# One turn for the last 64 keys of two heads, and one limit operation per beat

## The chip, the cores and the metric

The kernel runs on one core of one Trainium2 chip. The time is the device time in microseconds (us) of one execution; the kernel before took 1011.58 us (median of three runs, 1011.28 to 1013.16). In the text PE is TensorE, DVE is VectorE, ACT is ScalarE, POOL is GpSimd and SP is SyncE.

## The reference

```python
scores = scale * (q @ k.T)                      # 4 batches, 8 heads, 576 tokens, head size 64
thresh = scores.max(-1) - tau
scores = where(scores >= thresh, scores, -1e9)  # all far below a row's maximum is dropped
attn = exp(scores - scores.max(-1)); attn /= attn.sum(-1) + 1e-9
x = (attn @ v) put together over heads           # 2304 tokens x 512
x = (s * relu(x @ w_in)**2 + b) @ w_out          # first layer, hidden size 2048
h = x @ w_in2; x = (h * sigmoid(1.702 * h)) @ w_out2    # second layer
```

All is fp32. The kernel splits operands into a high and a low part of a faster fp32 format (fp32r) and adds the products of the parts.

## The kernel before

**Work and order.** The attention is cut into 160 tiles of query rows (128 or 96 rows each, 576 keys). Two tiles make a beat; there are 80 beats. Each engine has its own program, a loop over beats, with an order written out by hand; semaphores tie the engines together. From beat 15 on the steps of the first layer are woven in (one step per beat), and after the attention the steps and then the second layer (`TWINS`) follow alone.

**One beat.** PE computes the scores of the even tile (`scores_of`, four matmuls into one of two PSUM buffers), then those of the odd one. DVE makes the scaled row minimum (`row_max`, line 1045, which writes back the scaled scores and is followed by a read of the accumulator), then `limit_of` (line 1052: minimum plus tau, one column), per tile. In between DVE has `context_lo`, `invert_pair` (line 1059, the reciprocal of two row sums of the previous beat) and, from beat 16, `gated`. ACT computes exp (`exponent`, line 1269) as soon as the minimum is there. DVE then masks the even tile and the odd tile (`mask`, line 1071), with `gated_lo` (line 1108) between them in later beats. POOL adds eps (line 1547), and in its next beat scales both tiles (`norm`, line 1554). The scores buffer is free for PE again when its tile is masked.

**Turning the probabilities.** The products with the values need the keys on partitions. For the first six groups (32 tiles, beats 0 to 15) PE turns them two beats later: `turn_tile` has four transposes of 128 keys (line 769) into `y_ps[0]` or `y_ps[1]`, and one of the last 64 keys (line 773) into `y_ps[2]`, at column 0 for the even tile and column 128 for the odd one. ACT copies the four blocks (`copy_main`) and, once for both tiles, the last 64 keys (`copy_tails`, line 1301, 64 partitions). On PE a beat reads: scores even, turn even, scores odd, turn odd. For all later tiles DVE turns blocks of 32x32 (`turn`, line 1085) and DMAs put them in place; those are not touched by the change. `context_of` multiplies with the values: five chunks of 128 keys for each of two heads, where the fifth chunk has 64 keys and 64 rows of zeros.

**Ends of waits.** A tile's slot in `prob` (four slots) is free for `exponent` when PE has turned the tile. `context_hi` (line 1279, ACT) and `context_lo` (line 1093, DVE) split the result of `context_of` into its parts.

Of the kernel before, what the change touches and what calls it, by code (L numbers as in the profile page):

```python
# [9 lines left out]
ALU = mybir.AluOpType  # L10
ACT = mybir.ActivationFunctionType

P = 128
# [9 lines left out]
BATCH, HEADS_PER_BATCH, SEQ, HEAD_DIM = 4, 8, 576, 64  # L23
HEADS = BATCH * HEADS_PER_BATCH
PAIRS_PER_BATCH = HEADS_PER_BATCH // 2
# [2 lines left out]
BLK = 32  # L28
BLOCKS = SEQ // BLK
KEY_CHUNKS = 5  # L30
EPS = 1e-9
STATS = 8
PROBS = 4
# [19 lines left out]
PE_GROUPS = LONE_GROUPS + 2  # L53
FIRST_TILE = [2 * sum(TILES_PER_HEAD[n] for _, _, _, n in GROUPS_OF[:w]) for w in range(len(GROUPS_OF) + 1)]
FIRST_BEAT = [tile // 2 for tile in FIRST_TILE]
TILES = FIRST_TILE[-1]
# [163 lines left out]
B_FROM = 75  # L220
A_FROM = 88
A_APART = 4

# [28 lines left out]
PIECES = pieces_in_order()  # L254
# [56 lines left out]
VALUES = value_loads()  # L311
# [3 lines left out]
def tiles_of(beat, lag=0):  # L315
    return range(2 * beat - lag, 2 * beat - lag + 2)
# [41 lines left out]
def build(nc, q, k, v, consts_in, ident_in, slabs, twin_in, twin_out, out):  # L358
    ctx = ExitStack()
    with ctx:  # L360
# [7 lines left out]
        tau_in, s_c, b_c, eps_c, scale_c, tau_c, lower_c = (consts[:, n:n + 1] for n in range(7))  # L368
        ident = sbuf(ctx, "ident", [P, P])
# [64 lines left out]
        prob = sbuf(attn, "prob", [P, PROBS, SEQ])  # L434
        blocks = sbuf(attn, "blocks", [P, 2, BLOCKS, 2 * TILES_PER_HEAD[LONG], BLK])
        prob_t = sbuf(attn, "prob_t", [P, KEY_CHUNKS, 2 * LONG])
        neg_max = sbuf(attn, "neg_max", [P, STATS])
        limit = sbuf(attn, "limit", [P, STATS])
# [26 lines left out]
        y_ps = [ctx.enter_context(nc.psum_tensor(f"y_ps{n}", [P, 512], F32)) for n in range(GROUPS)]  # L465
# [6 lines left out]
        pads_zeroed = sem("pads_zeroed")  # L472
# [10 lines left out]
        max_ready = sem("max_ready")  # L483
# [50 lines left out]
        def turned_rows(w):  # L534

            return early_t if w < LONE_GROUPS and w % 2 == 1 else prob_t

        def turned_column(w, side, q):

            if w < LONE_GROUPS:  # L540
                return LONG * side + q
            return LONG * half_of(w) + SHORT * side + q
# [192 lines left out]
        def _(pe):  # L735
# [23 lines left out]
            def turn_tile(j):  # L759

                m = rows_of(j)
                w, side, t = TILE_AT[j]
                if j == 0:
                    pe.wait_ge(ident_loaded, 16)
                pe.wait_ge(normed, j + 1)
                if j >= 2:
                    pe.wait_ge(main_copied, j - 1)
                for c in range(KEY_CHUNKS - 1):
                    nc.tensor.transpose(y_ps[j % 2][:, c * P:c * P + m], prob[0:m, j % PROBS, c * P:(c + 1) * P],
                                        ident[0:m, 0:m])  # L770
                if side == 0 and j > 0:
                    pe.wait_ge(tail_copied, j // 2)
                nc.tensor.transpose(y_ps[2][0:64, side * P:side * P + m],
                                    prob[0:m, j % PROBS, (KEY_CHUNKS - 1) * P:SEQ], ident[0:m, 0:m]
                                    ).then_inc(rows_pe_turned, 1)

            def context_of(piece):

                w, n, _ = PIECES[piece]
                quads = (2 * n, 2 * n + 1) if is_long(w) else (0, 1, 2)  # L780
                if w >= PE_GROUPS:
                    for a in quads:
                        half = moved_into(w, a)
                        pe.wait_ge(moved[half][a], 64 * moves_before(w + 1, half, a))
                elif rides(piece):
                    pe.wait_ge(tail_copied, FIRST_BEAT[w + 1])
                    pe.wait_ge(main_copied, FIRST_TILE[w + 1])
                else:
                    pe.wait_ge(tail_copied, FIRST_BEAT[w] + n + 1)
                    pe.wait_ge(main_copied, FIRST_TILE[w] + 2 * n + 2)  # L790
                    pe.wait_ge(pads_zeroed, 2)
                    if piece > 0:
                        pe.wait_ge(context_lo_ready, piece)
                i = VALUE_OF[piece]
                pe.wait_ge(v_loaded[i % 2], 16 * (i // 2 + 1))
                for c in range(KEY_CHUNKS):
                    for side in range(2):
                        place = piece_bank(piece)[64 * side:64 * side + 64, :]
                        if w >= PE_GROUPS:
                            start = LONG * (n if is_long(w) else half_of(w))  # L800
                            rows = prob_t[:, c, start:start + LONG].rearrange("p (a s q) -> p a s q", a=len(quads),
                                                                              s=2)[:, :, side, :]
                            place = place.rearrange("p (a q) -> p a q", a=len(quads))
                        else:
                            start = turned_column(w, side, P * n)
                            rows = turned_rows(w)[:, c, start:start + piece_size(piece)]
                        mm = nc.tensor.matmul(place, v_sb[:, i % 2, side, c, :], rows,  # L807
                                              start=(c == 0), stop=(c == KEY_CHUNKS - 1))
                mm.then_inc(context_ready, 1)
# [208 lines left out]
        def _(dve):  # L1018
# [27 lines left out]
                                        accum_out=neg_max[0:m, j % STATS:j % STATS + 1]  # L1046
                                        ).then_inc(max_ready, 1)

            def limit_of(j):
                m, r = rows_of(j), j % STATS  # L1050
                dve.wait_ge(max_ready, j + 1)
                nc.vector.tensor_scalar(limit[0:m, r:r + 1], neg_max[0:m, r:r + 1], tau_c[0:m, :], None, ALU.add
                                        ).then_inc(limit_ready, 1)

            def invert_pair(j):
# [5 lines left out]
            def mask(j):  # L1061

                m, r = rows_of(j), j % STATS
                dve.wait_ge(limit_ready, j + 1)
                dve.wait_ge(exp_ready, j + 1)
                if j % 2 == 1 and riding(j // 2) is not None:
                    dve.wait_ge(context_hi_ready, riding(j // 2) + 1)
                if j % 2 == 0 and turn_due(j // 2 - MLP_FROM) is not None:
                    dve.wait_ge(x_ready, turns_by(j // 2 - MLP_FROM))
                p = prob[0:m, j % PROBS, :].rearrange("p (a n) -> p a n", a=2)  # L1070
                nc.vector.scalar_tensor_tensor(  # L1071
                    out=p, in0=scores[j % 2][0:m, :, 0:HALF], scalar=limit[0:m, r:r + 1],
                    in1=p, op0=ALU.is_le, op1=ALU.mult,
                    accum_out=row_sum[0:m, r:r + 1]).then_inc(masked, 1)
# [22 lines left out]
            def gated(n):  # L1097

                dve.wait_ge(gate_ready, n + 1)
                g = gate[:, n % 2, :]  # L1100
                nc.vector.scalar_tensor_tensor(out=g, in0=h_bank(n)[:, 0:TOK], scalar=s_c, in1=g, op0=ALU.mult,  # L1101
                                               op1=ALU.mult).then_inc(square_ready, 1)
# [80 lines left out]
            for beat in range(BEATS):  # L1183
                s = beat - MLP_FROM
                for j in tiles_of(beat):
                    if j < TILES:
                        row_max(j)
                        limit_of(j)
                    if j % 2 == 0 and alone(beat - 1) is not None:
                        context_lo(alone(beat - 1))  # L1190
                    if j % 2 == 0 and 0 <= j - 2 < TILES:
                        invert_pair(j - 2)
                    if j % 2 == 0 and s >= 1:
                        gated(s - 1)
                for j in tiles_of(beat):
                    if j < TILES:
                        mask(j)
                    if j % 2 == 0 and s >= 2:
                        gated_lo(s - 2)
                if riding(beat) is not None:  # L1200
                    context_lo(riding(beat))
                for j in tiles_of(beat, 2):
                    if PE_TILES <= j < TILES:
                        turn(j)
# [39 lines left out]
        def _(act_eng):  # L1244
# [48 lines left out]
            def copy_tails(j):  # L1293

                m = rows_of(j)
                w, _, t = TILE_AT[j]
                first, end = turned_column(w, 0, 0), 2 * turned_column(w, 1, 0) - turned_column(w, 0, 0)
                act_eng.wait_ge(rows_pe_turned, j + 2)
                if j == FIRST_TILE[w] and w >= 2:
                    act_eng.wait_ge(context_ready, TILES_PER_HEAD[LONG] * min(w - 1, LONE_GROUPS - 1))  # L1300
                nc.scalar.copy(turned_rows(w)[0:64, KEY_CHUNKS - 1, first:end].rearrange("p (s q) -> p s q", s=2)
                               [:, :, t * m:(t + 1) * m],
                               y_ps[2][0:64, 0:2 * P].rearrange("p (s q) -> p s q", s=2)[:, :, 0:m]
                               ).then_inc(tail_copied, 1)

            def slab_in_hi(n):

# [394 lines left out]
```

## Time and profile before

| what | value |
|---|---|
| median of three runs | 1011.58 us |
| the profiled execution | 1009.4 us, of which its span 1007.6 us |
| PE busy | 993.2 us (99%) |
| DVE, POOL, ACT busy | 798.0, 657.9, 606.6 us |
| TensorE clock granted | full over the span |

The profile counts an engine as busy while an instruction of it runs. Matmuls are pipelined and overlap, and their ends are modelled, so that a busy PE can still be a little late. In the timeline a name such as `scores<-k_hi,q_hl` is output and inputs; square brackets give the idle time of the engine ahead of the row and what ended it. Starts are us from the start of the span.

### The profile page before, as it was taken

How to read it: one execution, taken by the hardware profiler on the slowest of the kernel's cores; microseconds unless marked ns; L12 is line 12 of the kernel's file. 1: busy time of each engine (PE TensorE's matmuls, PEld its weight loads, DVE VectorE, ACT ScalarE, POOL GpSimd, SP SyncE). 2: the span in 40 equal slices, each digit the busy share in tenths (PEclk: the TensorE clock that was granted, in tenths of full speed). 3: DMA queues.
4: the chain of work that ended last, by engine and by line, in shares of the span. 5: the costliest groups of instructions: out<-in, count | busy, mean ns of one | idle time of the engine just before them, and what ended most of it. 6: DMA issues, size and time to landing. Idle time of an engine off the chain costs nothing.

```text
span 1007.6 us, 18212 instructions
## 1 busy us (share of the span) xinstructions
PE 993.2 (99%) x5922; PEld 895.4 (89%) x5922; DVE 798.0 (79%) x1749; ACT 606.6 (60%) x1124; POOL 657.9 (65%) x713
## 2 busy tenths in 40 slices
PE   8999999999999999999999999999999999999998
PEld 7788888888888888888899999998989989899897
DVE  7989999999999999999547766877767776566663
ACT  7877666666676666765555755555546555454443
POOL 6769997778788888886657775454544545445452
PEclk9999999999999999999999999999999999999999
DMA  7236776897977797778733541112122221222212
GB/s 216 73 116 187 209 204 189 218 239 213 228 199 191 204 246 190 209 179 217 211 106 126 185 150 32 63 42 85 44 82 87 102 84 46 81 87 102 84 48 79
DMA packets 97581, 142.50 MB, mean 141 GB/s; under 512 B 10320, under 2 KB 68944, under 8 KB 97488
## 3 DMA queue, kind: packets, MB, share of 16 engines
q1 hardware_dynamic: 97488, 141.34, 48.7%
q8 instruction: 49, 0.80, 0.3%
q14 instruction: 44, 0.36, 0.1%
HBM read 102.96 MB, written 4.72 MB: 107 GB/s over the span
## 4 chain that ended last, share of the span: by engine, by line
PE 85%; DVE 11%; issue 1%; DMA 1%; ACT 1%; POOL 0%; SPq 0%; DVEq 0%; POOLq 0%; ACTq 0%
PE shared L831 12%; PE y_ps L850 11%; PE shared L924 10%; PE y_ps L948 10%; PE scores L948 10%; PE scores L924 8%; PE scores L745 7%; PE scores L807 7%; PE scores L831 5%; PE y_ps L870 5%; DVE scores L1045 4%; DVE prob L1071 3%; PE scores L870 2%; DVE blocks L1085 1%; DMA k_raw<-k 1%
## 5 line engine op out<-in xcount | busy, mean ns | idle before, releaser
L1269 ACT ACTIVATE prob<-scores,neg_max 128x576 f32<-128x576 f32 (+1 forms) x160 | 118.6, 742 | 122.5 <-DVE scores L1045 122.4
L1614 POOL TENSOR_TENSOR a_sum_lo<-a_sum,a_hi 128x256 fp32r<-128x256 f32 x96 | 70.1, 740 | 182.5 <-DVE scores L1167 123.9
L1560 POOL TENSOR_TENSOR w_lo<-w_raw,win_hi 128x512 fp32r<-128x512 f32 x96 | 129.1, 1345 | 22.1 <-ACT win_hi L1311 17.7
L1567 POOL TENSOR_TENSOR w_lo<-w_raw,wout_hi 128x512 fp32r<-128x512 f32 x96 | 126.5, 1318 | 23.4 <-ACT wout_hi L1318 23.4
L1045 DVE TENSOR_SCALAR_CACHE_REDUCE scores<-scores,consts 128x576 f32<-128x576 f32 (+1 forms) x160 | 129.5, 809 | 13.1 <-PE scores L745 11.7
L1554 POOL TENSOR_SCALAR prob<-prob,row_inv 128x576 f32<-128x576 f32 (+1 forms) x160 | 126.8, 805 | 6.1 <-DVE row_inv L1059 5.7
L1071 DVE SCALAR_TENSOR_TENSOR prob<-scores,limit,prob 128x576 f32<-128x576 f32 (+1 forms) x160 | 128.1, 808 | 0.3
L831 PE MATMUL shared<-act_hi,win_hi 128*128 128x384 f32 x280 | 94.8, 339 | 1.1 <-DVE gate L1101 0.9
L831 PE MATMUL shared<-act_hi,w_lo 128*128 128x384 f32 x280 | 94.3, 337 | 0.0
L831 PE MATMUL shared<-act_lo,win_hi 128*128 128x384 f32 x280 | 93.9, 335 | 0.0
L1085 DVE STREAM_TRANSPOSE blocks<-prob 128x576 f32<-128x576 f32 (+1 forms) x128 | 91.4, 751 | 1.9 <-DMA prob_t<-blocks 1.7
L1108 DVE SCALAR_TENSOR_TENSOR g_lo<-gate,consts,g_hi 128x384 fp32r<-128x384 f32 x96 | 92.7, 966 | 0.2 <-ACT g_hi L1332 0.2
L1179 DVE TENSOR_TENSOR g_lo<-gate,g_hi 128x384 fp32r<-128x384 f32 x96 | 62.2, 650 | 33.4 <-ACT g_hi L1403 32.8
L745 PE MATMUL scores<-k_hi,q_hl 128*128 128x288 f32 (+1 forms) x320 | 76.6, 320 | 6.8 <-DVE prob L1071 6.2
L1332 ACT ACTIVATE g_hi<-gate,consts 128x384 fp32r<-128x384 f32 x96 | 59.0, 614 | 38.8 <-PE y_ps L870 27.9
L1395 ACT ACTIVATE gate<-scores 128x384 f32<-128x384 f32 x48 | 23.6, 492 | 94.9 <-DVE scores L1167 94.9
L1403 ACT CAST g_hi<-gate 128x384 fp32r<-128x384 f32 x96 | 49.2, 514 | 49.4 <-DVE gate L1174 40.0
L850 PE MATMUL y_ps<-wout_hi,g_hi 128*128 128x512 f32 x192 | 75.6, 394 | 0.0
L850 PE MATMUL y_ps<-wout_hi,g_lo 128*128 128x512 f32 x192 | 75.5, 393 | 0.0
L807 PE MATMUL scores<-prob_t,v_sb 128*64 128x192 f32 x800 | 73.8, 331 | 1.5 <-DVE prob L1071 0.9
L850 PE MATMUL y_ps<-w_lo,g_hi 128*128 128x512 f32 x192 | 74.9, 390 | 0.0
L1532 POOL TENSOR_TENSOR q_hl<-q_raw,q_hl 128x384 fp32r<-128x384 f32 (+1 forms) x51 | 49.0, 961 | 37.7 <-DVE g_lo L1108 31.2
(157 smaller groups left out, 2956.6 us busy)
## 6 DMA issues: line engine op xcount, KB each, us to landing
w_raw<-slabs SPq DMA_DIRECT2D x93, 512.0 KB, 4.2
a_raw<-twin_in SPq DMA_DIRECT2D x24, 512.0 KB, 4.6
o_raw<-twin_out SPq DMA_DIRECT2D x24, 512.0 KB, 3.6
prob_t<-blocks SPq DMA_DIRECT2D x96, 120.0 KB, 2.8
k_raw<-k SPq DMA_DIRECT2D x32, 288.0 KB, 4.6
prob_t<-blocks SPq DMA_DIRECT2D x96, 96.0 KB, 2.9
v_sb<-v SPq DMA_DIRECT2D x26, 320.0 KB, 4.3
q_raw<-q SPq DMA_DIRECT2D x40, 192.0 KB, 4.4
```

The costliest lines, as they stand in the source:

```text
L745: mm = nc.tensor.matmul(scores[j % 2][0:m, half, 0:HALF], q_hl[i % Q_RING][:, q0:q0 + m], part[key_slot(e)][:, half * HALF:(half + 1) * HALF],
L807: mm = nc.tensor.matmul(place, v_sb[:, i % 2, side, c, :], rows, start=(c == 0), stop=(c == KEY_CHUNKS - 1))
L831: mm = nc.tensor.matmul(bank[:, 0:TOK], wp[:, w], act_at(xp, c, tile * TOK, TOK), start=(c == 0 and k == 0), stop=(c == DC - 1 and k == 2))
L850: mm = nc.tensor.matmul(y_ps[g][:], gp[:, n % 2, toks], wp[:, :], start=(f == 0 and k == 0), stop=(f == SLABS - 1 and k == 2))
L924: mm = nc.tensor.matmul(twin_bank(x), wp, xp, start=(c == 0 and k == 0), stop=(c == 1 and k == 2))
L948: mm = nc.tensor.matmul(z_bank(tile, g), gp[:, i, toks], wp, start=(e == 0 and i < 2 and k == 0), stop=(e == TWIN_SLABS - 1 and i >= 2 and ...
L1045: nc.vector.tensor_scalar(place, place, scale_c[0:m, :], None, ALU.mult, ALU.min, accum_out=neg_max[0:m, j % STATS:j % STATS + 1]).then_in ...
L1071: nc.vector.scalar_tensor_tensor(out=p, in0=scores[j % 2][0:m, :, 0:HALF], scalar=limit[0:m, r:r + 1], in1=p, op0=ALU.is_le, op1=ALU.mult, ...
L1269: nc.scalar.activation(prob[0:m, j % PROBS, :].rearrange("p (a n) -> p a n", a=2), scores[j % 2][0:m, :, 0:HALF], ACT.Exp, bias=neg_max[0: ...
L1554: nc.gpsimd.tensor_scalar(prob[0:m, j % PROBS, :], prob[0:m, j % PROBS, :], row_inv[0:m, r:r + 1], 1.0, ALU.mult, ALU.mult).then_inc(norme ...
L1560: nc.gpsimd.tensor_tensor(in_of(w_lo, n), in_of(w_raw, n), win_hi[n % IN_HI][:].bitcast(F32), ALU.subtract).then_inc(win_lo_ready, 1)
L1567: nc.gpsimd.tensor_tensor(out_of(w_lo, n), out_of(w_raw, n), wout_hi[n % OUT_HI][:].bitcast(F32), ALU.subtract).then_inc(wout_lo_ready, 1)
```

## The change

For the tiles that PE turns, the odd head's keys are rolled by 64 columns on the host, so that its last 64 keys stand first in its slot of `prob`, right behind the last 64 of the even head in the slot before. One transpose over these 128 adjacent columns turns both; it stands behind the four transposes of the even tile and waits for the odd tile's `norm` too. The values of the odd head have their fifth chunk in partitions 64 to 127 and zeros in 0 to 63, and for the even head the reverse, so that both heads multiply the same turned columns. For the tiles that DVE turns, keys and values of the odd head are rolled alike. `copy_tails` copies 128 partitions by half the columns. And DVE makes both limits of a beat in one operation, after `gated` and both `row_max`.

```diff
-                    nc.tensor.transpose(y_ps[j % 2][:, c * P:c * P + m], prob[0:m, j % PROBS, c * P:(c + 1) * P],
-                                        ident[0:m, 0:m])
-                if side == 0 and j > 0:
-                    pe.wait_ge(tail_copied, j // 2)
-                nc.tensor.transpose(y_ps[2][0:64, side * P:side * P + m],
-                                    prob[0:m, j % PROBS, (KEY_CHUNKS - 1) * P:SEQ], ident[0:m, 0:m]
-                                    ).then_inc(rows_pe_turned, 1)
+                    mm = nc.tensor.transpose(y_ps[j % 2][:, c * P:c * P + m],
+                                             prob[0:m, j % PROBS, TAIL * side + c * P:TAIL * side + (c + 1) * P],
+                                             ident[0:m, 0:m])
+                if side == 0:
+                    pe.wait_ge(normed, j + 2)
+                    if j > 0:
+                        pe.wait_ge(tail_copied, j // 2)
+                    first = (j % PROBS + 1) * SEQ - TAIL
+                    mm = nc.tensor.transpose(y_ps[2][:, 0:m],
+                                             prob[0:m, :, :].rearrange("p a n -> p (a n)")[:, first:first + 2 * TAIL],
+                                             ident[0:m, 0:m])
+                mm.then_inc(rows_pe_turned, 1)
...
-                            start = turned_column(w, side, P * n)
+                            start = turned_column(w, side if c < KEY_CHUNKS - 1 else 0, P * n)
...
-            def limit_of(j):
+            def limit_pair(j):
                 m, r = rows_of(j), j % STATS
-                dve.wait_ge(max_ready, j + 1)
-                nc.vector.tensor_scalar(limit[0:m, r:r + 1], neg_max[0:m, r:r + 1], tau_c[0:m, :], None, ALU.add
+                dve.wait_ge(max_ready, j + 2)
+                nc.vector.tensor_scalar(limit[0:m, r:r + 2], neg_max[0:m, r:r + 2], tau_c[0:m, :], None, ALU.add
                                         ).then_inc(limit_ready, 1)
...
-                dve.wait_ge(limit_ready, j + 1)
+                dve.wait_ge(limit_ready, j // 2 + 1)
...
                     if j < TILES:
                         row_max(j)
-                        limit_of(j)
...
                     if j % 2 == 0 and s >= 1:
                         gated(s - 1)
+                if 2 * beat < TILES:
+                    limit_pair(2 * beat)
...
-                act_eng.wait_ge(rows_pe_turned, j + 2)
+                q0 = turned_column(w, 0, t * m)
+                act_eng.wait_ge(rows_pe_turned, j + 1)
+                if j == 0:
+                    act_eng.wait_ge(pads_zeroed, 2)
...
-                nc.scalar.copy(turned_rows(w)[0:64, KEY_CHUNKS - 1, first:end].rearrange("p (s q) -> p s q", s=2)
-                               [:, :, t * m:(t + 1) * m],
-                               y_ps[2][0:64, 0:2 * P].rearrange("p (s q) -> p s q", s=2)[:, :, 0:m]
-                               ).then_inc(tail_copied, 1)
+                nc.scalar.copy(turned_rows(w)[:, KEY_CHUNKS - 1, q0:q0 + m], y_ps[2][:, 0:m]).then_inc(tail_copied, 1)
...
+    keys[1::2] = np.roll(keys[1::2], TAIL, axis=2)
```

## Rows read from the trace of the kernel before

**Rows 1.** The chain that ended last, shares of the span by engine.

```profile
PE 85%; DVE 11%; issue 1%; DMA 1%; ACT 1%; POOL 0%; SPq 0%; DVEq 0%; POOLq 0%; ACTq 0%
```

**Rows 2.** Busy us by stretch: length, PE, PEld, DVE, ACT, POOL; clock, DMA share, GB/s.

```profile
14.00:67.00 53.00, 47.45 (x478) 41.39 (x479) 50.19 (x155) 45.00 (x94) 38.68 (x57) 1.00 0.35 109
...
83.00:132.00 49.00, 47.50 (x285) 41.38 (x282) 48.43 (x121) 33.42 (x62) 45.65 (x48) 1.00 0.70 197
132.00:184.00 52.00, 51.49 (x325) 45.30 (x325) 50.27 (x128) 33.13 (x61) 41.85 (x50) 1.00 0.74 204
184.00:485.00 301.00, 300.91 (x1950) 264.82 (x1948) 287.96 (x721) 198.27 (x374) 243.52 (x274) 1.00 0.81 210
```

**Rows 3.** Timeline of beat 7: start us, us, engine, line, operation, tiles.

```profile
34.87 0.83 DVE L1045 TENSOR_SCALAR_CACHE_REDUCE scores<-scores,consts 128x576 f32<-128x576 f32 x1 [0.15 <-PE scores L745]
...
35.48 0.43 PE L745 MATMUL scores<-k_lo,q_hl 128*128 128x288 f32 x2
35.58 0.29 ACT L1279 CAST act_hi<-shared 128x128 fp32r<-128x128 f32 x1
35.61 0.14 DVE L1045 DVE_READ_ACCUMULATOR scores<-scores,consts 128x1 f32 x1
...
35.78 0.21 DVE L1052 TENSOR_SCALAR limit<-neg_max,consts 128x1 f32<-128x1 f32 x1
35.91 0.28 DVE L1093 TENSOR_TENSOR act_lo<-shared,act_hi 128x128 fp32r<-128x128 f32 x1
...
36.11 0.16 DVE L1059 RECIPROCAL row_inv<-row_sum_eps 128x2 f32<-128x2 f32 x1
...
36.18 0.81 DVE L1045 TENSOR_SCALAR_CACHE_REDUCE scores<-scores,consts 128x576 f32<-128x576 f32 x1
...
36.49 0.37 ACT L1301 COPY early_t<-y_ps 64x256 f32<-64x256 f32 x1
...
37.09 0.21 DVE L1052 TENSOR_SCALAR limit<-neg_max,consts 128x1 f32<-128x1 f32 x1
37.22 0.81 DVE L1071 SCALAR_TENSOR_TENSOR prob<-scores,limit,prob 128x576 f32<-128x576 f32 x1
37.31 1.47 POOL L1554 TENSOR_SCALAR prob<-prob,row_inv 128x576 f32<-128x576 f32 x2
...
37.95 0.81 DVE L1071 SCALAR_TENSOR_TENSOR prob<-scores,limit,prob 128x576 f32<-128x576 f32 x1
...
38.09 0.54 PE L745 MATMUL scores<-k_hi,q_hl 128*128 128x288 f32 x2 [0.33 <-DVE prob L1071]
...
38.93 0.82 DVE L1045 TENSOR_SCALAR_CACHE_REDUCE scores<-scores,consts 128x576 f32<-128x576 f32 x1 [0.15 <-PE scores L745]
39.05 0.11 PEld L773 LDWEIGHTS y_ps<-ident,prob 128*64 128x64 f32 x1
```

**Rows 4.** Timeline of beat 3, the tail's transpose and the norm before it.

```profile
17.79 1.48 POOL L1554 TENSOR_SCALAR prob<-prob,row_inv 128x576 f32<-128x576 f32 x2
...
18.98 0.11 PEld L773 LDWEIGHTS y_ps<-ident,prob 128*64 128x64 f32 x1
...
19.93 0.83 DVE L1045 TENSOR_SCALAR_CACHE_REDUCE scores<-scores,consts 128x576 f32<-128x576 f32 x1
```

**Rows 5.** Timeline of beat 21, with the first layer woven in.

```profile
102.12 0.78 DVE L1045 TENSOR_SCALAR_CACHE_REDUCE scores<-scores,consts 96x576 f32<-96x576 f32 x1
...
103.13 0.15 DVE L1059 RECIPROCAL row_inv<-row_sum_eps 128x2 f32<-128x2 f32 x1
...
104.33 1.77 POOL L1554 TENSOR_SCALAR prob<-prob,row_inv 96x576 f32<-96x576 f32 x2
...
104.75 0.80 DVE L1071 SCALAR_TENSOR_TENSOR prob<-scores,limit,prob 96x576 f32<-96x576 f32 x1
...
105.48 1.02 DVE L1108 SCALAR_TENSOR_TENSOR g_lo<-gate,consts,g_hi 128x384 fp32r<-128x384 f32 x1
```

**Rows 6.** Groups by line and shape from 75 to 485 us: busy us, mean ns.

```profile
L1108 DVE SCALAR_TENSOR_TENSOR g_lo<-gate,consts,g_hi 128x384 fp32r<-128x384 f32 x63 | 43.9, 697 | 0.0
```

More of the change, by code:

```diff
@@ L30 @@
 KEY_CHUNKS = 5
+TAIL = 64
 EPS = 1e-9
@@ L1296, in copy_tails @@
                 w, _, t = TILE_AT[j]
-                first, end = turned_column(w, 0, 0), 2 * turned_column(w, 1, 0) - turned_column(w, 0, 0)
-                act_eng.wait_ge(rows_pe_turned, j + 2)
+                q0 = turned_column(w, 0, t * m)
+                act_eng.wait_ge(rows_pe_turned, j + 1)
+                if j == 0:
+                    act_eng.wait_ge(pads_zeroed, 2)
                 if j == FIRST_TILE[w] and w >= 2:
                     act_eng.wait_ge(context_ready, TILES_PER_HEAD[LONG] * min(w - 1, LONE_GROUPS - 1))
-                nc.scalar.copy(turned_rows(w)[0:64, KEY_CHUNKS - 1, first:end].rearrange("p (s q) -> p s q", s=2)
-                               [:, :, t * m:(t + 1) * m],
-                               y_ps[2][0:64, 0:2 * P].rearrange("p (s q) -> p s q", s=2)[:, :, 0:m]
-                               ).then_inc(tail_copied, 1)
+                nc.scalar.copy(turned_rows(w)[:, KEY_CHUNKS - 1, q0:q0 + m], y_ps[2][:, 0:m]).then_inc(tail_copied, 1)
             def slab_in_hi(n):
@@ L1676 @@
         queries.append(np.concatenate([cols, cols], axis=0))
-    keys = k_t.reshape(HEADS, HEAD_DIM, SEQ)
-    values = np.zeros((BATCH, HEADS_PER_BATCH, KEY_CHUNKS * P, HEAD_DIM), np.float32)
-    values[:, :, 0:SEQ, :] = v
-    values = values.reshape(BATCH, PAIRS_PER_BATCH, 2, KEY_CHUNKS, P, HEAD_DIM).transpose(0, 1, 4, 2, 3, 5)
-    values = np.stack([values[key] for key, _, _ in VALUES])
+    keys = k_t.reshape(HEADS, HEAD_DIM, SEQ).copy()
+    keys[1::2] = np.roll(keys[1::2], TAIL, axis=2)
+    values = np.zeros((2, BATCH, PAIRS_PER_BATCH, 2, KEY_CHUNKS * P, HEAD_DIM), np.float32)
+    values[:, :, :, :, 0:SEQ, :] = v.reshape(BATCH, PAIRS_PER_BATCH, 2, SEQ, HEAD_DIM)
+    values[1, :, :, 1, SEQ:SEQ + TAIL, :] = values[1, :, :, 1, SEQ - TAIL:SEQ, :]
+    values[1, :, :, 1, SEQ - TAIL:SEQ, :] = 0.0
+    values[0, :, :, 1, 0:SEQ, :] = np.roll(values[0, :, :, 1, 0:SEQ, :], TAIL, axis=2)
+    values = values.reshape(2, BATCH, PAIRS_PER_BATCH, 2, KEY_CHUNKS, P, HEAD_DIM).transpose(0, 1, 2, 5, 3, 4, 6)
+    values = np.stack([values[int(PIECES[first][0] < PE_GROUPS)][key] for key, first, _ in VALUES])
     first, second = slabs_of(moe_w_in, moe_w_out)
```

## The prediction, made before the changed kernel was run

> **What bounds the kernel now.** I read the chain of waits first, then busy time by stretch, then the timeline of single beats. The chain gives PE 85% and DVE 11% [rows 1]. The stretches place DVE's share: from 14 to 67 us (beats 2 to 14, attention alone) DVE is busy 50.19 of 53 us and PE 47.45; from 83 to 132 us (8 beats, with the first layer woven in) DVE is busy 48.43 of 49 us and PE is idle 1.50; from 132 to 184 us PE is idle 0.51; from 184 to 485 us only 0.09 of 301 us [rows 2]. Behind 485 us there is no line of the change. So DVE time is worth something up to about 184 us, and PE time behind that; a us won early moves all of PE's later work up by a us, because PE has no idle time later in which it could be lost.
>
> In an attention beat the loop is: mask of the even tile starts 37.22, PE's next scores start 38.09, the next row minimum 38.93, that is 1.71 us; then from the row minimum of the even tile at 34.87 to its mask at 37.22 are 2.35 us. Period 4.06 us, all through DVE [rows 3]. Within it: row minimum even 34.87, accumulator read to 35.75, limit 35.78, `act_lo` 35.91, reciprocal 36.11, row minimum odd 36.18, limit 37.09, mask 37.22 [rows 3].
>
> **The change part by part.**
>
> *One limit less.* The even tile's limit goes in all 80 beats. It starts 0.03 behind the end of the accumulator's read (35.75 to 35.78) and the next operation 0.13 behind its start, so `act_lo` starts 1.04 behind the row minimum [rows 3]. What follows a row minimum with no wait the trace does not show. From above: it starts when the read ends, at 0.88. From below: it starts with the read, at 0.74 (the odd mask starts 0.73 behind the even one, across a read, 37.22 to 37.95). In between: the limit (0.21 long) is followed after 0.13 and the reciprocal (0.16) after 0.07, so the next one starts 0.08 to 0.09 ahead of the end; by that it starts at 0.80 [rows 3]. I take 0.80, a saving of 0.24 (bounds 0.16 and 0.30).
>
> *What is late next.* The odd tile's row minimum would then start at 0.80 + 0.27 = 1.07 instead of 1.31. The odd tile's scores end at 35.91, 1.04 behind the even row minimum [rows 3], and the wait for them costs DVE some 0.03 more, as its own waits do (35.75 to 35.78 above). With the wider weight load below that is about 1.09. So in these beats 0.22 is saved, not 0.24, and no more than that even by the lower bound.
>
> *The pair's limit in front of the mask.* Before, the mask of the even tile waits for nothing that is late: it starts 0.13 behind the odd tile's limit, which it does not need. Now it needs this very operation: 0.21 of length and the 0.03 seen from the read's end to the limit's start [rows 3], 0.24 to 0.25, so 0.12 later. Below, nothing is lost if the hand-over costs no more than an ordinary start; above, 0.2 if it costs a good half again. I take 0.12. Net 0.10 a beat in attention beats, where DVE alone is late; where the odd row minimum waits for another engine, the beat gets 0.12 longer or, with slack at the mask, stays. The operation itself has two columns for one; nothing.
>
> The Trainium skill ("VectorE: DVE Perf Modes", The DRAIN you can't avoid) says that the next operation never starts before the pipe is empty, and that a semaphore between two operations therefore costs nothing extra. By that rule the mask would not be 0.12 later and a beat would gain 0.22. The rows disagree: an operation that does not wait starts 0.08 ahead of the end of the one before, one that waits 0.03 behind it [rows 3].
>
> *Attention beats 2 to 14.* ACT holds `act_lo` back in some: in beat 7 `act_hi` ends at 35.87, `act_lo` starts at 35.91 [rows 3], behind a cast of keys. By the order of the splits in the code this is so in beats 4, 6 and 7, and in beat 14 behind a cast of weights. There the removed limit gives nothing, and the mask's 0.12 is taken up, since the next even row minimum may be 0.12 later without `act_lo` being later. Seven beats (5, 8 to 13) gain 0.10: 0.7 us. Beats 2 and 3 have no `act_lo`; their odd row minimum waits for scores, so each may lose up to 0.12, and I take 0.15 for both.
>
> *The joint transpose.* Each pair loses one transpose, 16 in all, behind the odd tile's scores, where PE waits for the mask anyway (0.33 idle at 38.09 [rows 3]): worth nothing. The joint one has 128 columns for 64 in its weight load, about 0.03 longer, in front of the odd tile's scores: counted above. It now waits for the odd tile's `norm`; behind it on PE stand the odd tile's scores, and DVE waits for those. In beat 8 the norms end at 38.78 and the tail's load stands at 39.05: 0.27 of slack, in a beat where POOL had split keys [rows 3]. In beat 3 the norms end at 19.27 and the load stood at 18.98 [rows 4]: 0.29 too late. POOL's chain there starts behind a reciprocal that itself stands behind a removed limit and comes up to 0.24 earlier. I take 0.08 lost, once; bounds 0 and 0.3.
>
> *The copy of the tails.* It is 128 x 128 in place of 64 x 256 (0.37 [rows 3]); `act_hi` with 128 x 128 takes 0.29. ACT has idle time ahead of the odd exp, and the copy's wait ends a turn earlier. Nothing.
>
> Attention stretch: 0.7 - 0.15 - 0.08 = 0.5 us gained (bounds: 0.3 lost, 0.8 gained).
>
> *Woven beats.* Beat 16 waits for PE between its row minima: no gain, and the limit's 0.12 hides behind a later wait for `act_hi`. Beat 17 and the 8 beats from 83 to 132 us are DVE's throughput: row minimum 102.12, reciprocal 103.13, mask 104.75 [rows 5]. The row minimum is 0.78 here, so reciprocal, `gated` and odd minimum come 0.24 earlier, the mask 0.12: 9 x 0.12 = 1.1 us (bounds 9 x 0.04 and 9 x 0.18, the latter 1.6). PE has 1.50 us idle to give from 83 to 132 [rows 2], so 1.1 fits. `gated` being 0.24 earlier also ends PE's short waits for it.
>
> *Beats 25 to 33.* PE idles 0.51 us [rows 2], some of it for DMA. I take 0.4 (0.1 to 0.5). Behind that 0.09 is left: nothing.
>
> **The sum.** 0.5 + 1.1 + 0.4 = 2.0 us. The profiled execution of 1009.4 us (span 1007.6 and 1.8 around it) would come to 1007.4; it lies 2.2 under the median of the runs, which would come to 1009.6. The sum's own bounds are -0.3 + 0.4 + 0.1 = 0.2 and 0.8 + 1.6 + 0.5 = 2.9 us: 1011.4 to 1008.7.
>
> **Rivals.**
> 1. *The wait costs nothing (the skill's rule above as a mechanism here).* Beats gain 0.22 to 0.24: 7 x 0.22 - 0.08 = 1.5, then 1.5 (all of PE's idle time to 132 us) and 0.5: 3.5 us, 1008.1. Against it stand the starts in [rows 3].
> 2. *The end is elsewhere.* The odd row minimum waits in every attention beat for scores behind the joint transpose, and in the woven beats POOL, busy 45.65 of 49 us [rows 2], takes DVE's place through `norm`. For it: the scores end only 0.03 before the new start. Then 0.3 is lost first and perhaps 0.6 won later: 1011.3, no change that can be told from noise.
> 3. *Slower: DVE runs into POOL.* `gated_lo` takes 1.02 us beside a `norm` (104.33, 1.77 long; its two take 1.47 at 37.31) [rows 3, 5], and its mean over the woven beats is 0.697 [rows 6]. The mask moves against POOL's order, and `gated_lo` with it. If it fell beside the norms in every beat, a beat would be 0.32 longer on DVE: 9 x 0.32 = 2.9 lost before 132 us against 1.1 won, and behind that DVE, which has 301 - 287.96 = 13 us idle to 485 us [rows 2], would be late in some of its 46 beats, about 1.5 us more. With the 0.5 won: 2.8 us slower, 1014.4. It decides from the point where the mean rises by 0.12, what a beat wins. Against it: the move is only 0.1 to 0.2, and nothing says that it goes to the worse side.
>
> **How the numbers follow.** Forecast 0.57, rival 1 0.12, rival 2 0.18, rival 3 0.13. About 0.2% (2 us) is what a measurement here can tell from no change. The forecast lies on that edge and gives 0.33 to faster, 0.24 to the same; rival 1 goes to faster, rival 2 to the same, but for 0.01, rival 3 to slower. Faster 0.45, same 0.41, slower 0.14. The range reaches a little past rival 1 (PE's restarts after idle time may go too, which no term holds) and less than half of the way from rival 2 to rival 3: 1007.4 to 1012.6.
>
> **What would show it.** Right: line 1052's successor 80 times, the odd row minimum 1.07 to 1.12 behind the even one in beats 8 to 13 and its mask 0.24 to 0.25 behind the limit's start; a period of 3.96 there; beat 26 about 1.6 us earlier; from 184 us on all of PE's starts shifted by one constant, about 2 us. Wrong: the operation behind the even row minimum starts at 0.88 or waits; PE's joint load waits for POOL in more than beat 3; `gated_lo` above 0.75 in the mean; or PE's shift shrinks between 184 and 485 us.

## The result and the profile after

The changed kernel takes 1018.32 us (median of 6, 1017.13 to 1019.50) against 1010.63 (median of 6, 1009.16 to 1013.16) for the kernel before on the same chip: ratio 1.0082, interval 1.007 to 1.0094. It is 7.7 us slower. The forecast was 1009.6 us with a range to 1012.6; both are wrong, and so is the sign.

The profiled execution took 1019.28 us (span 1017.5 and 1.8 around it), 9.9 more than that of before. The chain that ended last, by engine, answers to [rows 1]: DVE's share went from 11% to 17%.

```profile
PE 74%; DVE 17%; DMA 3%; issue 2%; SPq 2%; ACT 1%; POOL 0%; DVEq 0%; POOLq 0%; ACTq 0%
```

Busy time in the same stretches as [rows 2] (length, then PE, PEld, DVE, ACT and POOL busy with their counts; clock, DMA share, GB/s):

```profile
14.00:67.00 53.00, 42.93 (x425) 38.02 (x425) 49.16 (x131) 39.52 (x86) 35.66 (x53) 0.97 0.35 108
...
83.00:132.00 49.00, 46.50 (x283) 40.03 (x282) 48.43 (x113) 34.30 (x64) 43.93 (x47) 1.00 0.66 191
132.00:184.00 52.00, 51.52 (x324) 45.46 (x323) 50.35 (x119) 33.31 (x60) 42.81 (x50) 1.00 0.68 191
184.00:485.00 301.00, 297.71 (x1916) 262.14 (x1915) 286.63 (x667) 198.27 (x370) 241.04 (x272) 1.00 0.80 208
```

DVE has fewer operations in every row and is hardly less busy: from 83 to 132 us 113 in place of 121, both times 48.43 us. So its operations got longer. PE's idle time from 184 to 485 us went from 0.09 to 3.29 us. Where the time was lost is seen in the starts of the even row minima, before and after: beat 2 14.86 and 14.87; beat 4 22.69 and 24.77; beat 8 38.93 and 41.25; beat 14 63.15 and 67.80; beat 34 184.54 and 190.10; beat 79 478.56 and 487.87. That is +2.1 in beats 2 and 3, +0.2 to beat 8, +2.3 from 8 to 14, +0.9 to beat 34, +3.8 to beat 79, and 0.6 after it.

The operation that got longer is the one that the change made. Before, a limit is one column, and never takes more than 217 ns; after, it is two columns (views of one line's instructions: count, ns of the shortest, median and longest, first and last start). The first fence is of before, the second of after; the last line of the second is the reciprocal, which had two columns before too.

```profile
L1052 DVE TENSOR_SCALAR limit<-neg_max,consts x160: 208/214/217, 7.9 to 481.2; 128x1 f32<-128x1 f32 x96, 96x1 f32<-96x1 f32 x64
```

```profile
L1062 DVE TENSOR_SCALAR limit<-neg_max,consts x80: 224/544/831, 8.9 to 490.2; 128x2 f32<-128x2 f32 x48, 96x2 f32<-96x2 f32 x32
...
L1069 DVE RECIPROCAL row_inv<-row_sum_eps x80: 119/158/166, 11.6 to 494.6; 128x2 f32<-128x2 f32 x80
```

Half as many limits take 40.8 us (mean 510 ns) where 160 took 34.0. The timeline of beat 9 after the change shows what one of the long ones does; it answers to beat 7 in [rows 3]:

```profile
45.69 0.83 DVE L1054 TENSOR_SCALAR_CACHE_REDUCE scores<-scores,consts 128x576 f32<-128x576 f32 x1
...
46.43 0.29 DVE L1103 TENSOR_TENSOR act_lo<-shared,act_hi 128x128 fp32r<-128x128 f32 x1
...
46.77 0.83 DVE L1054 TENSOR_SCALAR_CACHE_REDUCE scores<-scores,consts 128x576 f32<-128x576 f32 x1
46.89 1.47 POOL L1564 TENSOR_SCALAR prob<-prob,row_inv 128x576 f32<-128x576 f32 x2 [0.38 <-DVE row_inv L1069]
...
47.51 0.14 DVE L1054 DVE_READ_ACCUMULATOR scores<-scores,consts 128x1 f32 x1
...
47.69 0.69 DVE L1062 TENSOR_SCALAR limit<-neg_max,consts 128x2 f32<-128x2 f32 x1
...
48.42 0.82 DVE L1081 SCALAR_TENSOR_TENSOR prob<-scores,limit,prob 128x576 f32<-128x576 f32 x1
...
49.30 0.53 PE L749 MATMUL scores<-k_hi,q_hl 128*128 128x288 f32 x2 [0.89 <-DVE prob L1081]
...
50.13 0.82 DVE L1054 TENSOR_SCALAR_CACHE_REDUCE scores<-scores,consts 128x576 f32<-128x576 f32 x1
```

POOL's two norms run from 46.89 to 48.36. The limit starts at 47.69, inside them, and ends at 48.38, 0.02 behind their end. The mask follows at 48.42 and PE's next scores after that. The period is 4.44 us. In beat 9 of before a one-column limit runs inside the same norms and takes its 0.21:

```profile
44.48 1.47 POOL L1554 TENSOR_SCALAR prob<-prob,row_inv 128x576 f32<-128x576 f32 x2 [0.41 <-DVE row_inv L1059]
...
45.20 0.21 DVE L1052 TENSOR_SCALAR limit<-neg_max,consts 128x1 f32<-128x1 f32 x1
45.34 0.81 DVE L1071 SCALAR_TENSOR_TENSOR prob<-scores,limit,prob 128x576 f32<-128x576 f32 x1
```

So one more column turned an operation that passes POOL's into one that waits for it, and the wait is part of its duration in the profile, not idle time before it. Counted over the trace by single operations (a row of two norms is two): of the 80 limits of after, 51 start with more than 0.25 us of POOL's running operation to go, and all 51 end 0.020 to 0.029 us behind the end of that operation. So do all 57 that are longer than 0.3 us, behind one or another operation of POOL. Of the 160 limits of before 102 start with as much to go, and none is longer than 217 ns.

Not every operation of two columns does this. The reciprocal has one input and one output in SBUF too; in 63 of its 80 cases it starts with more than 0.25 us of POOL's operation to go (always a split there, never a norm, since the norms need its result), and it is never delayed. An example of after:

```profile
184.67 1.28 POOL L1577 TENSOR_TENSOR w_lo<-w_raw,wout_hi 128x512 fp32r<-128x512 f32 x1
184.90 0.16 DVE L1069 RECIPROCAL row_inv<-row_sum_eps 128x2 f32<-128x2 f32 x1
```

In beat 2 the same thing sets off a second loss. The limit waits for a key split on POOL, and PE idles 2.19 us before its scores at 18.54, where before it idled 1.44:

```profile
16.18 1.41 POOL L1550 TENSOR_TENSOR k_lo<-k_raw,k_hi 128x576 fp32r<-128x576 f32 x1
...
16.87 0.75 DVE L1062 TENSOR_SCALAR limit<-neg_max,consts 128x2 f32<-128x2 f32 x1
...
18.54 0.53 PE L749 MATMUL scores<-k_hi,q_hl 128*128 128x288 f32 x2 [2.19 <-DVE prob L1081]
```

Then PE's granted clock is 0.52 of full speed (the 1.2 GHz level) for 3.4 us. Two stretches of after:

```profile
16.00:19.00 3.00, 0.81 (x7) 0.57 (x5) 2.93 (x6) 2.82 (x7) 3.00 (x4) 1.00 1.00 333
19.40:22.80 3.40, 3.40 (x21) 3.05 (x21) 2.29 (x6) 1.58 (x4) 3.40 (x5) 0.52 0.92 337
```

Of the 6 runs of after three had a mean granted clock of 0.998 (mean 1019.16 us) and three of 1.000 (mean 1017.51). So executions with a clock stretch are some 1.65 us longer, and 6.9 us of the loss are there without one. The idle time alone does not decide it: pair_tt below idles 2.39 us in the same place, and its granted clock from 19 to 30 us was 1.00.

### The profile page after: what moved, and what is told of

It reads as the page before. It is cut to its first block, busy times and chain, and to the rows that moved or that the text cites. A ratio compares the mean times of both kernels' runs of the same rounds, so it can differ in the third digit from the quotient of the medians.

```text
span 1017.5 us, 18116 instructions
## 1 busy us (share of the span) xinstructions
PE 993.5 (98%) x5906; PEld 894.7 (88%) x5906; DVE 805.1 (79%) x1669; ACT 606.9 (60%) x1124; POOL 655.5 (64%) x713
## 4 chain that ended last, share of the span: by engine, by line
PE 74%; DVE 17%; DMA 3%; issue 2%; SPq 2%; ACT 1%; POOL 0%; DVEq 0%; POOLq 0%; ACTq 0%
PE shared L933 10%; PE scores L957 10%; PE y_ps L957 10%; PE shared L840 8%; PE scores L933 8%; PE y_ps L859 7%; DVE scores L1054 6%; PE scores L816 5%; PE scores L840 5%; PE scores L749 5%; PE y_ps L879 5%; DVE prob L1081 3%; DVE blocks L1095 3%; DMA prob_t<-blocks 2%; DVE g_lo L1118 2%
## 5 line engine op out<-in xcount | busy, mean ns | idle before, releaser
L1118 DVE SCALAR_TENSOR_TENSOR g_lo<-gate,consts,g_hi 128x384 fp32r<-128x384 f32 x96 | 88.8, 925 | 0.2 <-ACT g_hi L1342 0.2
L1542 POOL TENSOR_TENSOR q_hl<-q_raw,q_hl 128x384 fp32r<-128x384 f32 (+1 forms) x51 | 49.0, 960 | 40.8 <-DVE g_lo L1118 36.2
```

## The experiments

Three theories went into the first four runs. P: the two-column limit waits for POOL's running operation. T: the joint transposes, with their wait for `norm` and their wider copy. O: the late place of the limit, between the odd row minimum and the even mask, is itself what costs. The second four tell the two forms of P apart (narrow: only the operation with one tensor input and two columns; wide: also one with two tensors in SBUF) and try what the first four pointed to. "Before" was 1010.34 us in the first group (23 runs) and 1009.99 in the second (11 runs).

**tails_only.** The change without the pair's limit:

```diff
-                nc.vector.tensor_scalar(limit[0:m, r:r + 2], neg_max[0:m, r:r + 2], tau_c[0:m, :], None, ALU.add
+                nc.vector.tensor_scalar(limit[0:m, r:r + 1], neg_max[0:m, r:r + 1], tau_c[0:m, :], None, ALU.add
...
                         row_max(j)
+                        limit_of(j)
...
-                if 2 * beat < TILES:
-                    limit_pair(2 * beat)
```

> The joint transpose and the value layout of the change, with the two one-column limits at their old places. Theory P (the two-column limit waits for whatever POOL is running: in the changed kernel it takes 0.22 to 0.83 us and ends 0.02 us behind POOL's operation, where the one-column one took 0.21): the loss is gone, 1009.5 to 1012. Theory T (the joint transpose makes PE late, which in beat 2 idles 2.2 us and then runs 3.4 us at the lower clock): most of the 8 us stay, 1014 to 1018. Theory O (the loss comes from the late place of the limits, in front of the mask): 1010 to 1012, as P.

Measured 1011.17 us, ratio 1.0009 (0.9998 to 1.002). Even row minima: beat 3 18.74, beat 4 23.09, beat 14 63.54, so 0.38 is lost in beat 3 (from 3.97 to 4.35) and nothing from there to beat 14. There the joint load waits for `norm`, which the odd tail's load of before had not done:

```profile
19.43 0.14 PEld L781 LDWEIGHTS y_ps<-ident,prob 128*128 128x128 f32 x1 [0.30 <-POOL prob L1562]
```

T holds a few tenths of a us in the early beats of this execution, not 8 us. The joint transposes may have a second cost: 6 of these 12 runs have a mean granted clock of 0.998 (mean 1012.80 us) and 6 have 1.000 (1009.87), against 2 and 21 for before (1011.19 and 1010.22). So the 0.8 us between the medians lies in the runs with a low clock; where those have it no trace shows.

**pair_only.** The kernel before with the pair's limit of the change and nothing else of it; the tails are turned as before.

> The two-column limit of the change alone, tails turned as before. P: 1016 to 1018.5, the limit's mean near 0.5 us and its end at the end of POOL's operation. T: 1010 to 1012. O: 1016 to 1018, as P.

Measured 1018.06 us, ratio 1.0078 (1.0065 to 1.0091): the whole loss. Its 80 limits have a mean of 509 ns, its beats 4, 14 and 34 begin at 24.79, 67.82 and 190.09, all within 0.02 us of after, and its profiled run has the clock stretch too (0.52 from 19.4 to 22.8 us). P and O both gave this range.

**two_late.** The change with two one-column limits in the place of the pair's:

```diff
-                if 2 * beat < TILES:
-                    limit_pair(2 * beat)
+                for j in tiles_of(beat):
+                    if j < TILES:
+                        limit_of(j)
```

> The whole change, but the limit of two columns is two limits of one column each at the same late place. P: each takes 0.21 us whatever POOL does; a beat gains 0.30 at the even row minimum (one operation and its wait) and loses 0.26 in front of the mask, so about nothing: 1009 to 1012. O: the mask stays as late as the place makes it, 1015 to 1018. T: 1014 to 1018.

Measured 1006.54 us, ratio 0.9961 (0.9949 to 0.9973), 3.8 us faster than before. The period from beat 8 to 14 is (61.98 - 39.12) / 6 = 3.81 us, against 4.04 before and 4.43 after. Beat 9 of this kernel:

```profile
44.01 0.82 DVE L1054 TENSOR_SCALAR_CACHE_REDUCE scores<-scores,consts 128x576 f32<-128x576 f32 x1
...
44.13 1.47 POOL L1564 TENSOR_SCALAR prob<-prob,row_inv 128x576 f32<-128x576 f32 x2
...
44.75 0.39 DVE L1061 TENSOR_SCALAR limit<-neg_max,consts 128x1 f32<-128x1 f32 x2
...
45.06 0.81 DVE L1080 SCALAR_TENSOR_TENSOR prob<-scores,limit,prob 128x576 f32<-128x576 f32 x1
```

The first limit starts with the read of the odd row minimum (44.75), since the even minimum has long been there, and both run inside the norms (44.13 to 45.60) without delay. O falls: same order, same number of columns in all, one more instruction, and the loss is a gain. What differs from the changed kernel is one instruction of two columns against two of one; with it the even mask no longer needs the younger result, and wide_limits below, where no such wait changes, tells the two apart. P's range missed as well: I expected 1009 to 1012, with 0.26 lost in front of the mask. The mask in fact comes 1.05 behind the odd row minimum (44.01 to 45.06), as in before (1.04), so the 0.24 won at the odd row minimum is kept.

**pair_on_act.** The change with the pair's limit on ACT:

```diff
+                nc.scalar.activation(limit[0:m, r:r + 2], neg_max[0:m, r:r + 2], ACT.Identity,
+                                     bias=tau_c[0:m, :]).then_inc(limit_ready, 1)
```

> The whole change, but ACT makes the limit of two columns, in front of the odd tile's exp, as an Identity activation with tau as bias. P: DVE is as in the forecast of 2 us gained, without POOL in the way: 1007.5 to 1010.5, the mask 0.25 to 0.3 us behind the read of the odd row minimum. O: the mask still waits for the pair's limit, 1014 to 1018. T: 1014 to 1018.

Measured 1011.49 us, ratio 1.0014 (1.0005 to 1.0022). It removes nearly all of the loss, but I expected 1007.5 to 1010.5, and it missed. The operation takes 283 to 298 ns in all 80 cases, whatever POOL does; but it starts 0.17 behind the read's start, is 0.30 long, and its mask comes 1.25 behind the odd row minimum (44.49 to 45.74) for 1.04 before:

```profile
45.41 0.30 ACT L1281 ACTIVATE limit<-neg_max,consts 128x2 f32<-128x2 f32 x1 [0.17 <-DVE scores L1054]
45.74 0.82 DVE L1074 SCALAR_TENSOR_TENSOR prob<-scores,limit,prob 128x576 f32<-128x576 f32 x1 [0.36 <-ACT limit L1281]
```

That takes up what the removed limit gave: period 4.02.

**wide_limits.** The kernel before with every one of its 160 limits made two columns wide, in its old place (the second column is padding that nothing reads):

```diff
-        neg_max = sbuf(attn, "neg_max", [P, STATS])
-        limit = sbuf(attn, "limit", [P, STATS])
+        neg_max = sbuf(attn, "neg_max", [P, STATS, 2])
+        limit = sbuf(attn, "limit", [P, STATS, 2])
...
-                nc.vector.tensor_scalar(limit[0:m, r:r + 1], neg_max[0:m, r:r + 1], tau_c[0:m, :], None, ALU.add
+                nc.vector.tensor_scalar(limit[0:m, r, :], neg_max[0:m, r, :], tau_c[0:m, :], None, ALU.add
```

> The kernel before with each of its 160 limits two columns wide (the second column is a zero plus tau and is never read). Places and count are those of before, only the width differs. P (two columns of fp32 in SBUF with a scalar, as against one, wait for POOL's running operation): the mean rises from 0.21 to 0.4 to 0.55, 1015 to 1030. A theory by place (the late position alone hurts): 1009 to 1012.

Measured 1035.65 us, ratio 1.0252 (1.0239 to 1.0265). That is 25.7 us slower, above the range I gave. Nothing is moved and no wait between the engines is changed; one unused column is added, and one memset with its wait at the very start. Of its 160 limits 82 start with more than 0.25 us of POOL's operation to go, and all 82 end 0.020 to 0.028 us behind it. First its group of limits (busy us, mean ns, idle us before), then rows of one beat:

```profile
L1055 DVE TENSOR_SCALAR limit<-neg_max,consts 128x2 f32<-128x2 f32 (+1 forms) x160 | 79.4, 496 | 5.7
```

```profile
52.16 1.00 POOL L1535 TENSOR_TENSOR q_hl<-q_raw,q_hl 128x384 fp32r<-128x384 f32 x1 [0.32 <-ACT q_hl L1256]
...
52.63 0.56 DVE L1055 TENSOR_SCALAR limit<-neg_max,consts 128x2 f32<-128x2 f32 x1
...
53.55 1.48 POOL L1557 TENSOR_SCALAR prob<-prob,row_inv 128x576 f32<-128x576 f32 x2 [0.39 <-DVE row_inv L1062]
...
54.27 0.23 DVE L1055 TENSOR_SCALAR limit<-neg_max,consts 128x2 f32<-128x2 f32 x1
```

The even limit ends at 53.19, 0.03 behind POOL's split (53.16); the odd one of the same beat takes 0.23 in the middle of the norms. That row stands for two operations, and the first would end at 53.55 + 0.74 = 54.29, right when the limit comes (54.27). So it is the single operation that is running that has to end, and a limit that comes as it ends can slip in ahead of the next. In 11 beats here the limit starts 0.002 to 0.005 us ahead of the second norm and takes 0.22 to 0.23. Where it comes a little later it waits the next one out: at 104.88 it starts 0.04 behind the start of a split and takes 1.28.

**pair_tt.** The change with `tau` read as a second tensor of two columns, not as a scalar:

```diff
-                nc.vector.tensor_scalar(limit[0:m, r:r + 2], neg_max[0:m, r:r + 2], tau_c[0:m, :], None, ALU.add
+                nc.vector.tensor_tensor(limit[0:m, r:r + 2], neg_max[0:m, r:r + 2], tau_pair[0:m, :], ALU.add
```

> The whole change, but the pair's limit as TENSOR_TENSOR with a tile of two taus in place of TENSOR_SCALAR. P in its wide form (any operation that takes two streams out of SBUF at once meets POOL; gated_lo with two SBUF inputs has shown 0.61 to 1.02): mean near 0.5, 1016 to 1019. P in its narrow form (only the one-input operation's double rate meets POOL): each 0.2 to 0.25, 1006 to 1009.

Measured 1015.89 us, ratio 1.006 (1.0046 to 1.0074). Its limits are 156 ns at the shortest and 982 at the longest, mean 430. One of them, beside the norms that end at 47.03:

```profile
45.56 1.47 POOL L1569 TENSOR_SCALAR prob<-prob,row_inv 128x576 f32<-128x576 f32 x2 [0.38 <-DVE row_inv L1074]
...
46.35 0.68 DVE L1067 TENSOR_TENSOR limit<-neg_max,tau_pair 128x2 f32<-128x2 f32 x1
```

It ends at 47.03. Of its 80 limits 48 start with more than 0.25 us of POOL's operation to go, and all 48 end 0.002 to 0.020 us behind it. The wide form of P holds: this operation with two inputs in SBUF waits for POOL as well. The time lies just under that form's range of 1016 to 1019.

**spread.** What the runs pointed to: the kernel before with its one-column limits kept on DVE but taken away from behind their own row minima, the even one to behind `gated`, the odd one to between the masks.

```diff
                         row_max(j)
-                        limit_of(j)
...
                         gated(s - 1)
+                    if j % 2 == 0 and j < TILES:
+                        limit_of(j)
...
+                    if j % 2 == 0 and j < TILES:
+                        limit_of(j + 1)
```

> The same spread limits with the tails turned as before the change (no joint transpose). S: within 0.5 us of the run with joint transposes, as these alone gave 1011.2 against 1010.3; if the joint transpose costs by its wait for the second norm in beats 2 and 3, this one is 0.2 to 1 us faster than that.

Measured 1004.86 us, ratio 0.9946 (0.9934 to 0.9958): 5.1 us faster than before, and the lowest median of all. Period (60.83 - 38.94) / 6 = 3.65 us. Its DVE in one beat:

```profile
43.57 0.20 DVE L1052 TENSOR_SCALAR limit<-neg_max,consts 128x1 f32<-128x1 f32 x1
43.68 0.82 DVE L1045 TENSOR_SCALAR_CACHE_REDUCE scores<-scores,consts 128x576 f32<-128x576 f32 x1
...
44.41 0.81 DVE L1071 SCALAR_TENSOR_TENSOR prob<-scores,limit,prob 128x576 f32<-128x576 f32 x1
```

The even mask starts 0.73 behind the odd row minimum, with its read, since nothing that it needs is young. PE is busy 49.01 us from 14 to 67 us in place of 47.45.

**spread_tails.** The same on top of the joint transposes of the change.

> Joint transposes, one-column limits, the even one behind gated, the odd one between the two masks, so that neither stands behind a wait for its own row minimum or in front of the mask that needs it. Theory S (DVE's waits are what is won): in attention beats the even mask starts 0.74 behind the odd row minimum in place of 1.05, at 0.13 more ahead of that minimum: 0.18 less than the two late limits' 3.82; in beats with a split of keys ACT ends the wait and nothing is won; 1005 to 1006.2. Theory E (behind beat 19 PE is the bound, and only attention counts; the odd mask then waits for its exp): 1006.2 to 1007, no better than the two late limits' 1006.5.

Measured 1005.28 us, ratio 0.9951 (0.994 to 0.9963): in the range of S, below that of E. Between this and spread there is nothing that these runs can tell: the joint transposes are worth nothing here, as forecast.

## Why the prediction was wrong

The step that failed is one sentence of the sum: "The operation itself has two columns for one; nothing." I took the duration of the two-column limit from the one-column one and gave it no bound from above. The nearest rows of before spoke for both ends: the reciprocal, 128 x 2, starts in 60 of its 80 cases with more than 0.25 us of POOL's operation to go and never takes more than 158 ns; `gated_lo` takes 1.02 us beside a norm [rows 5], where its shortest is 0.61. With the second as the upper end (a limit can wait for a whole norm, 0.74) the slower rival would have had this place too. What the runs showed in place of "nothing": 0.51 us in the mean and 0.69 in beats 8 to 13, against 0.21.

By the steps:

- *One limit less.* Right in kind, with the saving at its upper bound of 0.30: the next operation starts with the accumulator's read, 0.74 behind the row minimum (45.69 to 46.43), not 0.80. The odd row minimum comes 1.08 behind the even one, inside the 1.07 to 1.12 forecast.
- *The pair's limit in front of the mask.* The hand-over itself was right: the mask starts 0.04 behind the limit's end. But the limit is 0.69 long for 0.21, so the mask comes 1.65 behind the odd row minimum (46.77 to 48.42), where the forecast has 0.91 + 0.25 = 1.16. A beat is 4.44 and not 3.96. In beats 8 to 13 it is the same each time: the norms start 0.25 behind the reciprocal's start, the first ends 1.00 and the second 1.72 to 1.73 behind it; the limit comes 1.04 to 1.05 behind it, just too late for the gap between the two.
- *Attention stretch.* Forecast 0.5 won; measured 4.6 lost between beats 2 and 14: 2.3 in beats 8 to 14, six times 0.39, and 2.1 in beats 2 and 3, of which some 1.65 goes with the clock (by the difference between the runs), which no term held; 0.2 was lost in between.
- *Joint transpose.* Right in kind: worth nothing, with a wait in beat 3. Its size was 0.38 in the run that shows it alone, above the forecast 0.08 and its bound of 0.3. That its runs have the low clock more often than those of before was in no term.
- *Woven beats.* Forecast 1.5 won to 184 us; measured 0.9 lost from beat 14 to 34. The limits there are long too (median 704 ns from 83 to 132 us), but `gated_lo` pays for a part of it: it takes 608 to 615 ns in all 16 cases between 83 and 184 us, I think since the limit in front of it has already waited the norms out.
- *Behind 184 us.* "Nothing" was true only for a gain. PE is the bound there, with 13 us of slack on DVE in before, yet 3.8 us are lost: 7 times PE waits for a late mask. In the answer of the waits (us in total, times, longest):

```profile
PE scores L816 <- DVE prob L1081: 2.8, 7, 0.7
```

- *Rivals.* Rival 3 had the sign, the mechanism (DVE meets POOL) and 0.13 of the chance, but put it on the wrong operation: on `gated_lo`, whose mean in fact fell from 690 to 643 ns from 184 us on. Rival 1 is out, since needing a fresh result does cost (0.91 to 0.92 behind a row minimum against 0.74). Rival 2 is out, since the odd row minimum comes 1.07 to 1.08 behind the even one in beats 8 to 13 and waits for no scores.

The Trainium skill has a mechanism that fits. Its page "SBUF — State Buffer", SBUF: two separate sides, says that DVE in one of its two-port modes, or with two inputs in SBUF (then only against a GpSimd operation that reads SBUF), shares a port pair with GpSimd as an exclusive lock, held for a whole instruction, and that the other "fully blocks". The runs agree for DVE's side: limits end 0.02 to 0.03 behind POOL's operation, and pair_tt shows the second case. The Trainium skill's "VectorE: DVE Perf Modes", What auto-detection actually checks, says that where firmware enables it the two-port mode is taken by itself when a single source and the destination are in SBUF, with outermost sizes other than one that are even or equal. Here the two-column limit waits and the one-column one does not, as by that rule; the reciprocal of two columns does not wait either, which the shape alone does not explain. That it is this lock I infer from the ends of operations; no run here took the ports themselves apart, a limit kept outside SBUF was not tried, and what sets the reciprocal apart stays open.

The remaining doubt is small. Of the 3.29 us that PE idles from 184 to 485 us the waits for the mask name 2.8 and one for a DMA 0.3; in the tails_only execution one wait for a DMA of 0.9 us fell in the same stretch, so some tenths there are scatter. The 0.6 us behind beat 79 I did not take apart.

## What to carry to other kernels

Before merging two small operations on VectorE into one, look at what runs on GpSimd at that moment: the merged one may wait for it, and the wait hides in its duration. A row with a duration far above the shortest of its kind (here 1.02 against 0.61) is worth a question for every operation that a change makes wider. And where an operation only waits for a fresh result, look at moving it away from the result: here the kernel with all 160 limits, spread, won 5.1 us, while merging them lost 7.7 and handing them to ACT won nothing.

## What the runs showed of the hardware

- A two-column `tensor_scalar` in SBUF takes 0.23 us alone and up to 831 ns (1317 in wide_limits) beside POOL; one column takes 189 to 218 ns in every run, beside POOL or not, and a two-column reciprocal at most 167.
- The operation behind a row minimum starts with the read of its accumulator (0.74) if it waits for nothing young, and at 0.91 to 0.92 if it needs the minimum. Each such dependence costs DVE 0.17 us, more than the 0.13 from a limit's start to the next operation's.
- PE's idle time in beat 2 and the clock after it: 2.19 us (after) and 2.41 us (pair_only) were followed by 3.4 us at 0.52 of full speed, the 1.2 GHz level; 2.39 us (pair_tt) and 1.63 us (tails_only) were not, with a granted clock of 1.00 from 18 to 23 us. So its length does not tell the two apart; what does stays open.
